# Windowed attention into two MoE-style layers: mask and row maxima of a sequence's first tile by one VectorE instruction a head, and three reorderings

## What is computed

```python
scores = (q @ k.T) / sqrt(64)            # per sequence and head
keep = (key < 4) | ((0 <= pos - key) & (pos - key < 128))
a = exp(scores_masked - max); a = a / (sum(a) + 1e-9)
x = (a @ v) laid out as 1536 tokens x 512
h = x @ w_in                             # 512 -> 1024
solu = h * softmax(h)
ln = (solu - mean) / sqrt(var + 1e-6) * g_ln
x2 = ln @ w_out                          # 1024 -> 512
out = relu(x2 @ w2_in) ** 2 @ w2_out     # 512 -> 2048 -> 512
```

## Time and profile before

| | us (share of the span) |
|---|---|
| median of 3 runs | 483.87 |
| the profiled execution | 483.68 |
| its span, first to last instruction | 481.7 |
| PE busy | 472.0 (98%) |
| DVE busy | 280.4 (58%) |
| ACT busy | 213.1 (44%) |
| POOL busy | 102.6 (21%) |
| granted TensorE clock, mean over the span | 1.000 of full speed (2.4 GHz) |

### The profile page before, as it was taken

How to read it: one execution, slowest core, us unless ns; L and a number is a source line. 1 busy time by engine, 2 the same in 40 slices (tenths; PEclk the granted TensorE clock), 3 DMA queues, 4 the chain that set the end, 5 groups by cost and what they waited for, 6 DMA issues and landing times.

```text
span 481.7 us, 7313 instructions
## 1 busy us (share of the span) xinstructions
PE 472.0 (98%) x2636; PEld 383.0 (80%) x2636; DVE 280.4 (58%) x490; ACT 213.1 (44%) x562; POOL 102.6 (21%) x153
## 2 busy tenths in 40 slices
PE   7999999999999999999999999999999999999997
PEld 6667787877788888878888888888888888888885
DVE  4999889899989888767755354322222233222232
ACT  4787876665777666242324253222222232222222
POOL 2365423320321232739930000000000000000000
PEclk9999999999999999999999999999999999999999
DMA  8921437766478424497300000200000020000002
GB/s 213 324 88 46 144 100 197 229 167 191 112 199 202 111 57 120 119 258 234 90 0 0 1 1 1 87 0 0 0 0 0 0 87 1 0 0 1 0 1 87
DMA packets 51670, 41.80 MB, mean 87 GB/s; under 512 B 28024, under 2 KB 37496, under 8 KB 51128
## 3 DMA queue, kind: packets, MB, share of 16 engines
q1 hardware_dynamic: 51032, 40.74, 29.8%
q10 hardware_dynamic: 608, 0.66, 0.5%
HBM read 30.38 MB, written 11.01 MB: 86 GB/s over the span
## 4 chain that ended last, share of the span: by engine, by line
PE 92%; DVE 3%; POOL 2%; DMA 1%; ACT 1%; issue 0%; ACTq 0%; DVEq 0%; POOLq 0%
PE score_ps L1619 27%; PE h_ps L1633 14%; PE w_ps L1460 13%; PE h_ps L1420 12%; PE w_ps L1633 7%; PE wt_ps L1633 7%; PE o_ps L1386 4%; PE score_ps L1352 2%; PE wt_ps L1352 2%; PE h_ps L1437 1%; PE wt_ps L1363 1%; DMA x2T<-qT 1%; PE o_ps L1407 1%; POOL pT_own L552 1%; POOL pT_earlier L556 1%; DVE prob L1061 1%
## 5 line engine op out<-in xcount | busy, mean ns | idle before, releaser
L1619 PE MATMUL score_ps<-x2T_hi,w2in_hi 128*128 (+1 forms) x192 | 74.8, 389 | 0.0
L1619 PE MATMUL score_ps<-x2T_hi,w2in_lo 128*128 (+1 forms) x192 | 74.7, 389 | 0.0
L1619 PE MATMUL score_ps<-x2T_lo,w2in_hi 128*128 (+1 forms) x192 | 74.7, 389 | 0.0
L1279 DVE TENSOR_TENSOR e<-e 128x512 f32<-128x512 f32 x24 | 17.9, 744 | 82.0 <-ACT e L937 82.0
L1279 DVE TENSOR_TENSOR sq<-relu 128x512 f32<-128x512 f32 x24 | 17.2, 718 | 76.9 <-ACT relu L937 76.8
L937 ACT ACTIVATE relu<-score_ps 128x512 f32<-128x512 f32 x24 | 14.3, 597 | 90.4 <-PE score_ps L1619 90.4
L937 ACT ACTIVATE e<-score_ps 128x512 f32<-128x512 f32 x24 | 14.4, 599 | 89.7 <-PE score_ps L1619 89.7
L1619 PEld LDWEIGHTS score_ps<-x2T_lo,w2in_hi 128*128 128x128 f32 x192 | 36.1, 188 | 7.5
L1619 PEld LDWEIGHTS score_ps<-x2T_hi,w2in_lo 128*128 128x128 f32 x192 | 36.0, 188 | 7.4
L1619 PEld LDWEIGHTS score_ps<-x2T_hi,w2in_hi 128*128 128x128 f32 x192 | 36.0, 187 | 7.4
L712 ACT ACTIVATE prob<-sm,nbias 128x132 f32<-128x132 f32 (+1 forms) x96 | 37.7, 394 | 0.8
(11 more groups left out here) (189 smaller groups left out, 1096.5 us busy)
## 6 DMA issues: line engine op xcount, KB each, us to landing
u_dram<-uT SPq DMA_DIRECT2D x18, 256.0 KB, 3.3
lnT_raw<-u_dram SPq DMA_DIRECT2D x36, 128.0 KB, 2.8
w2in<-w_in SPq DMA_DIRECT2D x4, 1024.0 KB, 5.3
w2out<-w_out SPq DMA_DIRECT2D x8, 512.0 KB, 10.2
V<-v SPq DMA_DIRECT2D x12, 256.0 KB, 3.3
x2T<-x_dram SPq DMA_DIRECT2D x12, 256.0 KB, 4.7
x_dram<-x SPq DMA_DIRECT2D x44, 64.0 KB, 2.2
k_raw<-kT SPq DMA_DIRECT2D x20, 132.0 KB, 2.8
```

Source lines behind the costliest of these rows:

```text
L1279: nc.vector.tensor_tensor(sq[f % 2], relu[f % 2], relu[f % 2], ALU.mult).then_inc(sq_ready, 1)
L1619: done = mm(h2_ps[f % 2], ws[:, c, fs], xs[:, c, bass.ts(blk, BLK)], start=(c == 0 and i == 0), stop=(c == MC - 1 and i == 2))
```

## The change

It has four parts.

1. For tiles 0 and 6, the addition of the mask and the maximum of four heads (two instructions) become four instructions, one a head, each of which adds the mask and keeps the running maximum. `nmax` is then not negated, so `bias` scales by -SCALE for these tiles, and it waits for `merged` instead of `maxed`.
2. On DVE at the start, `round_w_in(0)` and `round_w_in(1)` stand behind `normalize_p(0, 0)` and `normalize_p(0, 1)` instead of ahead of them, and `split_w_in(1)` stands behind `row_max(1, 1)` instead of ahead of `merge(1, 0)`.
3. On PE at the start, the first `keep_warm` has 13 matmuls instead of 16, and `hidden_0(3, False)` stands ahead of `hidden_0(1, True)`.
4. In step 2 alone, `normalize_p(4, 1)` stands ahead of `hidden_max(3, 1)`.

```diff
             def bias(n, g):
                 hs = slice(g * HG, (g + 1) * HG)
-                act.wait_ge(maxed, GROUPS * n + g + 1)
-                nc.scalar.activation(nbias[:, hs], nmax[:, hs], ACT.Copy, scale=SCALE).then_inc(biased, 1)
+                if alone(n):
+                    act.wait_ge(merged, merges(n, (g + 1) * PAIRS // GROUPS))
+                else:
+                    act.wait_ge(maxed, GROUPS * merged_before(n) + g + 1)
+                nc.scalar.activation(nbias[:, hs], nmax[:, hs], ACT.Copy, scale=-SCALE if alone(n) else SCALE
+                                     ).then_inc(biased, 1)
...
                         if since(n, 1):
                             dve.wait_ge(exped, H * n)
-                        nc.vector.tensor_tensor(
-                            sm[:, g * HG:(g + 1) * HG, main(n)].rearrange("p (c j) k -> p j c k", j=2),
-                            score_banks(n, p)[:, :, 0:2 * P].rearrange("p j (c k) -> p j c k", k=P),
-                            alone_mask[:, :].unsqueeze(1).unsqueeze(1).to_broadcast([P, 2, HG // 2, P]), ALU.add
-                            ).then_inc(merged, 1)
+                            dve.wait_ge(biased, GROUPS * n)
+                        for slot in range((p - 1) * 2, (p + 1) * 2):
+                            c, j = slot % HG // 2, slot % 2
+                            last = nc.vector.tensor_tensor_reduce(
+                                sm[:, slot, main(n)], score_banks(n, p)[:, j, c * P:(c + 1) * P], alone_mask[:, :],
+                                1.0, LOWEST, ALU.add, ALU.max, nmax[:, slot:slot + 1])
+                        last.then_inc(merged, 1)
...
                 normalize_p(t + 2, 0)
                 hidden_max(n, 0)
+                if t == EARLY:
+                    normalize_p(t + 2, 1)
                 hidden_max(n, 1)
                 hidden_max_all(n)
-                normalize_p(t + 2, 1)
+                if t > EARLY:
+                    normalize_p(t + 2, 1)
...
             row_max(0, 1)
+            normalize_p(0, 0)
             round_w_in(0)
-            normalize_p(0, 0)
+            normalize_p(0, 1)
             round_w_in(1)
-            normalize_p(0, 1)
             split_w_in(0)
-            split_w_in(1)
             merge(1, 0)
...
             row_max(1, 1)
+            split_w_in(1)
             normalize_p(1, 0)
...
-            keep_warm(16)
+            keep_warm(13)
...
             hidden_0(0, True)
+            hidden_0(3, False)
             hidden_0(1, True)
-            hidden_0(3, False)
             hidden_0(2, True)
```

More of the change, by code:

```diff
@@ L26 @@
 MASKED = -1e9 / SCALE
+LOWEST = -3e38
 TPB = S // P
@@ L981, in merge @@
                     if p % 2:
-                        g = p // 2
                         dve.wait_ge(scored, PAIRS * n + p + 1)
@@ L1003, in row_max @@
                     dve.wait_ge(sinks_hidden, GROUPS * (n // TPB) + g + 1)
-                dve.wait_ge(merged, merges(n, (g + 1) * PAIRS // GROUPS))
-                nc.vector.tensor_reduce(nmax[:, hs], sm[:, hs, seen(n)], AX_X, ALU.max, negate=True
-                                        ).then_inc(maxed, 1)
+                if not alone(n):
+                    dve.wait_ge(merged, merges(n, (g + 1) * PAIRS // GROUPS))
+                    nc.vector.tensor_reduce(nmax[:, hs], sm[:, hs, seen(n)], AX_X, ALU.max, negate=True
+                                            ).then_inc(maxed, 1)
             def hidden_max(t, half):
```

## The result

| | before | changed |
|---|---|---|
| median of 14 executions each, us | 484.28 | 487.98 |
| lowest and highest | 483.83 and 485.92 | 486.10 and 489.95 |
| profiled execution, us | 483.68 | 486.34 |
| its span | 481.7 | 484.4 |

The account below looks back on a forecast made before the run. The prediction took the chain of waits, 92% of it PE, to bound the kernel. From the profiled 483.68 us it summed 0 (tile 0), +1.2 (split_w_in(1)), +1.1 (normalize_p(4, 1)) and +0.3 (tile 6) to 486.3, range 484.2 to 487.6.

Parts of the forecast that it names:

- the two large terms: Moving split_w_in(1) behind row_max(1, 1) in tile 1, +1.2 us, and normalize_p(4, 1) ahead of hidden_max(3, 1) in step 2, +1.1.
- Tile 0: nothing: Tile 0: maxima come 0.2 us earlier, but PE and ACT wait for landings of v and k, so no gain.
- The third rival: Only the way through prob counts: tile 0 passes on 0.25 us, step 2 gains 0.7; 482.7 us, chance 0.05.
- A group of four heads: 1.24 us: New mask-and-maximum instructions on DVE: 0.31 us a head, 1.24 a group, between 1.1 and 1.88.
- The rival of slow reads: Accumulator reads wait for their instruction: a group 1.88 us, tile 0 costs 0.3, tile 6 1.0; 487.3 us, chance 0.09.
- split_w_in(1): +1.2: Tile 1: the subtraction on DVE takes turns with POOL, making prob and the transposes late by 1.2 us (+0.6 to +1.5).
- its first branch: Tile 1, POOL first: w_lo runs from 21.65 to 22.8 us, and prob ends at 24.0 to 24.4 instead of 22.89.
- normalize_p(4, 1): +1.1: Step 2: transposes 0.7 us earlier, but the sinks' copy and sink_values 1.12 later, with a PE pause of about 2 us.
- Tile 6: +0.3: Tile 6: four heads make split_xT 0.5 us later, part comes back; net +0.3, between +0.1 and +1.0.
- The clock: nothing: The sum had no clock term; a rival put nine slower matmuls after the start's longer pauses, +1.7 us, 488.0, chance 0.03.
- the prediction's own second term: Step 2: normalize_p(4, 1) ahead of hidden_max(3, 1) costs +1.1 us, with a PE pause of about 2 us before sink_values.
- this rival: PE's clock falls in the start's longer pauses: nine matmuls cost 1.7 us more, 488.0 us; chance 0.03.

Follow-up runs that it names:

- e11: The changed kernel with part 4 undone (normalize_p(4, 1) again behind hidden_max(3, 1) in step 2): median 485.12 us.
- e3: The kernel before with part 4 alone (normalize_p(4, 1) ahead of hidden_max(3, 1) in step 2): median 486.79 us.
- e6: The changed kernel with split_w_in(1) back at its old place on DVE, ahead of tile 1's merges: median 486.42 us.
- e4: The changed kernel with POOL building and rounding the first sequence's v sink rows ahead of its part of w_in, not behind: median 489.18 us.
- e8: The changed kernel with seven matmuls for nothing on PE, by mistake ahead of sink_values(3), a step before the pause: median 489.27 us.
- e1: The kernel before with part 1 alone (mask and maximum by one instruction a head in tiles 0 and 6): median 483.54 us.
- e2: The kernel before with parts 2 and 3 alone (the start's order on DVE and PE, 13 matmuls for 16): median 485.70 us.
- e5: The changed kernel with ACT's copies of p's and the sinks' transposes ahead of hidden_exp(3) and hidden_sum(3) in step 2: median 485.75 us.
- e7: The kernel before with parts 1 and 4, and ACT's copies for the transposes ahead of hidden_exp(3); the start's order is old: median 484.88 us.
- e9: The changed kernel with seven matmuls for nothing on PE directly ahead of sink_values(4), in the 1.90 us pause: median 486.04 us.
- e12: The kernel of e10 with eleven instead of nine warm-up matmuls ahead of q: median 483.68 us.
- e10: The kernel before with part 1; in step 2 two output-projection products between p's transposes, and hidden_sum behind ACT's copies: median 483.93 us.

## Why the forecast was right, and where it was not

Taken as a difference from 483.68, the forecast was +2.6 us, with a range of +0.5 to +3.9. The medians differ by 3.70 and the profiled executions by 2.66. The direction and the two large terms came out as worked out. The largest miss is the clock behind the pause of step 2, which the sum put at nothing.

- **Tile 0: nothing.** Wrong, it is -0.42. The step that failed is "PE cannot use it: its loads for `values(0, 0)` waited until 12.77 us for v from memory". That wait is one of PE's weight loads, beside three busy matmuls of `keep_warm`. In the changed kernel the same 0.48 stands there, with nothing that ended it:

```profile
13.16 0.45 PEld L1397 LDWEIGHTS o_ps<-pT_earlier,V 128*64 128x64 f32 x8 [0.48 <-issue]
```

  What ended PE's own wait in tile 0 was `prob`, at 11.37 in the kernel before (the row is above, under the result); the prediction didn't look at that row. Nor are the landings fixed times: `values(0, 0)` started at 12.06 in e11's profile, and in e3's PE did wait for v, until 13.31, so there are executions in which v decides. The third rival had this part right, and its size (0.25) too small.
- **A group of four heads: 1.24 us.** It is 0.85. A head's slot is 0.21, not 0.24, and the accumulator's read costs no slot, not 0.07. The rival of slow reads is out. The estimate by the rule of the Trainium skill (VectorE: DVE Perf Modes, the section on the TRN2 errata) was 1.03 without the reads; the 0.85 measured is below it, so the measurement decides.
- **split_w_in(1): +1.2.** It is +1.19 by e6 alone, and +1.23 to +1.33 with the rest of the start's order. By the rows the mechanism was the one named, in its first branch: POOL's multiplication was ahead by 0.02, and POOL and DVE took turns. No experiment took the turns away by itself; e4's rows put about half of the delay of `prob` on the turns.
- **normalize_p(4, 1): +1.1.** It is +1.09. Transposes 0.73 earlier behind B (0.66 against 1.39), a pause of 1.90 where "about 2 us" was forecast, and the sinks' copy that ends it are all in the rows. What was left out is what the pause does to the clock (below).
- **Tile 6: +0.3.** It is -0.14. The step that failed is "Four heads instead of one addition make `split_xT` 0.63 - 0.1 = 0.5 later": DVE's `xT_lo` came only 0.09 later behind the first instruction of the group (2.69 us against 2.60), since a group costs 0.24 more than the addition and not 0.63, and 0.14 of it fell into a gap of DVE ahead of `xT_lo`. PE's `hidden(5)` came 0.10 later behind C, and the pause of 0.2 ahead of the scores at the step's end, which the prediction named, is gone.
- **The clock: nothing.** It is +1.9 in ten executions of fourteen. The prediction put the danger at the pauses of the start and gave it 0.03, for 1.7 us. The step that failed is the argument against it, "PE paused 0.93 us in step 2 and went on at full rate": that is the old pause, and the prediction's own second term made one of 2 us out of it. That this rival's time, 488.0, is almost the median is luck: it adds one fall of the clock to the forecast, but in another place.

Summed up, the measured terms are -0.42 + 1.33 + 1.09 - 0.14 = +1.86 on 484.28, or 486.1, and the clock adds 1.9 in ten executions of fourteen. The forecast of 486.3 met the profiled execution (486.34) by errors that cancel: tile 0 and tile 6 too dear by 0.86, q's landing by chance 0.82 later. The median of 487.98 lies above 487.6, the range's upper end; the kernel before, timed beside it, had 484.28 and not 483.68, and as a difference 3.70 is inside.

## What to carry to other kernels

Ask at each wait on PE's critical path what stands in front of the releasing instruction in its engine's stream; here an earlier `prob` made ACT's queue late, and the pause only moved and doubled. A wait in the row of weight loads is no wait of PE while its matmuls are busy. Price a pause of PE that grows not only by its length: look at the granted clock of several executions, and fill it if nothing shortens it.

## What the runs showed of the hardware

- **The clock behind a pause.** All kernels with a pause of 1.90 us in that place (the changed one, e3, e4, e6, e8) had a lower clock in 32 of 49 executions; those whose longest pause there was 0.93 us or less, or was filled (e1, e2, e5, e7, e9 to e12), in 2 of 92, and the kernel before in none of the 99 beside the experiments. It costs 1 to 2 us, and in e3 it was at 1.2 GHz for some 3.5 us. The 1.2 GHz was seen in the profiles of e3, e4 and e8; the cost is the difference between the groups of e3, e6 and the changed kernel (1.0, 1.1 and 1.9 by medians). Why some executions escape, and why two fell without such a pause, is open.
- **The start's half rate is not in the granted clock.** The clock's column says 1.00 from the first microsecond, while the first nine matmuls take 0.44 us each, and the first scores of e10 and of e4 1.23 instead of 0.71. There are values between: 0.96 in e6, 0.92 in e8, 0.81 in e12 and 0.79 in e7, and there S to A is longer than the 4.94 of the changed kernel by as much (0.25, 0.20, 0.10, 0.07). In e4 it is 0.83 longer and in e10 2.01, so e10's long start, which e12's expectation calls the only one, is the longest of six. The durations tell it, the column doesn't. The kernel before takes 483.2 to 484.9 us in most executions and 485.1 to 486.9 in some; that this is the same thing was not shown.
- **Turns between DVE and POOL go both ways.** `w_lo` took 2.09 us for 1.21 beside POOL's multiplication (e2: 2.08), and POOL's cast then 1.49 for 0.61. In e4, where POOL's four subtractions ran beside it, `w_lo` kept its 1.22 and those took 4.26 for 2.82. Even `z_eps`, four numbers a partition, took 0.57 for 0.16.
